# Attention, the order within a step: TensorE turns four tiles before the next scores, VectorE copies them before it adds the bias

## The chip, the core and the metric

The kernel runs on one core of one Trainium2 chip. The metric is the device time in microseconds of one execution; lower is better. The kernel before took 1315.04 us, the median of three executions (1312.54, 1315.04 and 1316.11).

## The reference, cut to what matters

```python
def _attn_ref(q, k, v, w1, b1, w2):          # q, k, v: 4 x 8 x 576 x 64, float32
    scores = np.matmul(q, k.transpose(0, 1, 3, 2)) / np.sqrt(D)
    ...                                       # bias: a table 576 x 576 for each of 8 heads
    scores = scores + bias.transpose(2, 0, 1)[None, :, :, :]
    scores = scores - np.max(scores, axis=-1, keepdims=True)
    attn = np.exp(scores)
    attn = attn / (np.sum(attn, axis=-1, keepdims=True) + 1e-09)
    return np.matmul(attn, v)
```

Behind it stand a dense layer (2304 tokens, 512 to 2048 to 512, with h - tanh(h) between) and a layer of 8 experts, of which each token goes to the one with the largest gate. All tensors are float32.

## The kernel before, in words

The program has five blocks, one after the other: `bias_tables`, `attention`, `dense_layer`, `routing` and `experts`. Only `attention` is touched.

It works on 16 pairs of heads, g = 0 to 15. A head has 576 queries, in QT = 5 tiles: t = 0 to 3 have 128 rows, t = 4 has 64. The list `STEPS` holds all (g, t) in order, with five steps ahead of the first pair and five behind the last; n = 5 g + t numbers a pair's tiles. Each engine goes through the same list with its own instructions, written out by hand. A step does several jobs on different tiles at once, and semaphores hold the engines together. In step n:

- TensorE (from line 396): `scores` of tile n+1 (line 341) multiplies q by k for both heads c = 0 and 1, as three products of split numbers (high by high, high by low, low by high), in two halves of 288 keys: 12 matmuls. Then four transposes of the probabilities of tile n into the bank `pt_a` (line 404, through `turn_prob`, line 355), then products with v (`values_main`, lines 407 to 410: one slot in step 4, and of the pair before one slot, two slots and one slot in steps 0, 1 and 2, none in step 3), then four transposes into `pt_b` (line 415). Then come transposes of the next pair's q and k (line 430; steps 0 to 3), in step 2 the last 64 queries' products with v (line 423), in steps 3 and 4 transposes of the output `o_sb` (line 439), and one last transpose of tile n, `mid`, into the bank `misc` (line 444).
- VectorE (from line 518): `add_bias` of tile n+1 for both heads (line 487): it reads the scores and the bias, writes the negated sum `neg` and its row minimum `negmax`. Then the copy of `pt_a` into `prob_t` (line 529), then the low parts of the next pair's k and q (lines 536 and 539), and, for the pair before: the reciprocal of the sums in step 1, two copies into `o_sb` in step 2 (lines 551 and 555), the scaling into `x_sb` in steps 3 and 4 (line 511).
- ScalarE (from line 459): the exponential of tile n+1 of head 0 (line 454), the copy of `pt_b` (line 472), the copy of `mid` (line 474), the high parts of the next pair's k and q (line 479), the exponential of tile n+1 of head 1.
- SP loads q, k, v and the bias, and stores `x_sb` to `x_dram`.

Each engine works strictly in the order of its list. What matters here: `scores` of tile n+1 waits until both bias additions of tile n have read its banks (line 343); the `pt_a` transposes of tile n wait for that tile's exponential of head 0 (`prob_done[0]`, line 401) and for VectorE's copy of tile n-1 (`pta_read`, line 403); the `pt_b` transposes wait for the exponential of head 1 (line 412). An exponential waits for its own `add_bias` (line 451). The `o_sb` copy of the remainder waits for ScalarE's `mid` copy (line 554).

Of the kernel before, what the change touches and what calls it, by code (L numbers as in the profile page):

```python
# [30 lines left out]
QT = -(-S // P)  # L31
# [13 lines left out]
def rows(t):  # L45

    return P if t < QT - 1 else LAST
# [149 lines left out]
def attention(nc, bias_dram, q, k, v, ident, x_dram):  # L197
# [6 lines left out]
    with ExitStack() as ctx:  # L204
# [58 lines left out]
        def q_at(t):  # L263

            return 0 if t == QT - 1 else LAST + t * P
# [14 lines left out]
        def real(g):  # L280
            return 0 <= g < PAIRS_A
# [3 lines left out]
        with nc.Block() as block:  # L285
# [49 lines left out]
            @block.tensor  # L335
            def _(pe):
                def scores(g, t):
                    n = g * QT + t
                    if t == 0 or NEEDED[t] > NEEDED[t - 1]:
                        pe.wait_ge(lo_done, NP * g + NEEDED[t])  # L340
                    for c in range(2):
                        if n:
                            pe.wait_ge(neg_done[c], n)
                    cols = slice(q_at(t), q_at(t) + P)
                    for half in range(2):
                        keys = slice(half * HALF, (half + 1) * HALF)
                        for i, (a, b) in enumerate(((q_hi, k_hi), (q_hi, k_lo), (q_lo, k_hi))):
                            for c in range(2):
                                part = slice(c * D, (c + 1) * D)
                                last = nc.tensor.matmul(score[c][:, half, 0:HALF], a[g % 2][part, cols], b[g % 2][part, keys],  # L350
                                                        start=i == 0, stop=i == 2)
                                if half and i == 2:
                                    last.then_inc(score_done[c], 1)

                def turn_prob(bank, at, n, j):
                    m = rows(n % QT)
                    src = prob[n % 2][0:m, :, :].rearrange("p c s -> p (c s)")[:, j * P:(j + 1) * P]
                    return nc.tensor.transpose(bank[:, at:at + m], src, id_sb[0:m, 0:m])

                def values(g, slot, o, at, queries):  # L360

                    j_a, j_b = (slot, MID + 1 + slot) if slot < MID else (MID, MID)
                    for c, j in ((0, j_a), (1, j_b)):
                        keys = slice(0, P) if j != MID else slice(c * D, (c + 1) * D)
                        last = nc.tensor.matmul(o[c * D:(c + 1) * D, at:at + queries.stop - queries.start],  # L365
                                                v_nat[g % NV][keys, j, :], prob_t[g % 2][keys, j, queries],
                                                start=slot == 0, stop=slot == MID)
                    return last

                def values_main(g, slots):  # L370
                    if 0 in slots:
                        pe.wait_ge(v_in[g % NV], 16 * (g // NV + 1))
                        pe.wait_ge(pta_read, QT * g + QT - 1)
                        pe.wait_ge(ptb_read, QT * g + QT - 1)
                        pe.wait_ge(mid_read, QT * g + QT - 1)
                        if g:
                            pe.wait_ge(o_read, g)
                    for slot in slots:
                        last = values(g, slot, o_acc, 0, slice(0, MAIN))
                    if MID in slots:  # L380
                        last.then_inc(o_done, 1)

                def misc_free(g, t):

                    pg, pt = (g, t - 1) if t else (g - 1, QT - 1)
                    if real(pg):
                        pe.wait_ge(mid_read, QT * pg + pt + 1)
                    if pt < NP and real(pg + 1):
                        pe.wait_ge(lo_done, NP * (pg + 1) + pt + 1)
                    if pt == 2 and real(pg - 1):  # L390
                        pe.wait_ge(rem_read, pg)
                    if pt >= 3 and real(pg - 1):
                        pe.wait_ge(x_done, 2 * (pg - 1) + pt - 2)

                pe.wait_ge(id_in, 16)
                for g, t in STEPS:
                    n = g * QT + t
                    if real((n + 1) // QT):
                        scores((n + 1) // QT, (n + 1) % QT)
                    if real(g):  # L400
                        pe.wait_ge(prob_done[0], n + 1)
                        if n:
                            pe.wait_ge(pta_read, n)
                        for j in range(MID):
                            last = turn_prob(pt_a, j * P, n, j)
                        last.then_inc(pta_done, 1)
                    if t == QT - 1 and real(g):
                        values_main(g, (0,))
                    if t < 3 and real(g - 1):
                        values_main(g - 1, ((1,), (2, 3), (4,))[t])  # L410
                    if real(g):
                        pe.wait_ge(prob_done[1], n + 1)
                        if n:
                            pe.wait_ge(ptb_read, n)
                        for j in range(MID + 1, KTP):
                            last = turn_prob(pt_b, (j - MID - 1) * P, n, j)
                        last.then_inc(ptb_done, 1)
                    misc_free(g, t)
                    if t == 2 and real(g - 1):
                        pe.wait_ge(pta_read, QT * g)  # L420
                        pe.wait_ge(ptb_read, QT * g)
                        pe.wait_ge(mid_read, QT * g)
                        for slot in range(MID + 1):
                            last = values(g - 1, slot, misc, REM, slice(MAIN, S))
                        last.then_inc(rem_done, 1)
                    if t < NP and real(g + 1):
                        if t == 0:
                            pe.wait_ge(qk_in[(g + 1) % NQK], 128 * ((g + 1) // NQK + 1))
                        at = P
                        for x, tile, m in PIECES[t]:  # L430
                            nat = (k_nat if x == "k" else q_nat)[(g + 1) % NQK]
                            last = nc.tensor.transpose(misc[:, at:at + m], nat[0:m, tile, :], id_sb[0:m, 0:m])
                            at += m
                        last.then_inc(prep_done, 1)
                    if t in TURNED and real(g - 1):
                        pe.wait_ge(o_read, g)
                        if t == 4:
                            pe.wait_ge(rem_read, g)
                        for tile, at in TURNED[t]:
                            m = rows(tile)  # L440
                            last = nc.tensor.transpose(misc[0:m, at:at + P], o_sb[:, tile * P:tile * P + m], id_sb[:, :])
                        last.then_inc(turn_done, 1)
                    if real(g):
                        turn_prob(misc, 0, n, MID).then_inc(mid_done, 1)
# [41 lines left out]
            def _(dve):  # L486
# [31 lines left out]
                for g, t in STEPS:  # L518
                    n = g * QT + t
                    m = rows(t)  # L520
                    if real((n + 1) // QT):
                        add_bias(n + 1, 0)
                        add_bias(n + 1, 1)
                    if real(g):
                        if t == 0 and g >= 2:
                            dve.wait_ge(rem_done, g - 1)
                        dve.wait_ge(pta_done, n + 1)
                        src = pt_a[:, :].rearrange("p (k m) -> p k m", m=P)
                        nc.vector.tensor_copy(prob_t[g % 2][:, 0:MID, t * P:t * P + m], src[:, :, 0:m]).then_inc(pta_read, 1)
                    if t < NP and real(g + 1):  # L530
                        i = (g + 1) % 2
                        dve.wait_ge(hi_done, NP * (g + 1) + t + 1)
# [1046 lines left out]
```

## Time and profile before

| | us |
|---|---|
| median of three executions | 1315.04 |
| the profiled execution | 1314.88 |
| its span, first to last instruction | 1312.9 |
| TensorE matmul, busy | 1078.8 (82%) |
| VectorE, busy | 710.6 (54%) |
| ScalarE, busy | 567.5 (43%) |
| bias additions, line 496, 160 of them, busy | 113.9 |
| exponentials, line 454, 160 of them, busy | 124.2 |

The profile is of one execution. The hardware profiler's times are microseconds from the first instruction unless marked ns. PE is TensorE's matmuls, PEld its weight loads, DVE VectorE, ACT ScalarE. A busy time can contain time in which a matmul only drains, since ends of matmuls are modelled: a matmul's start after the one before it says more than its duration. The attention's first instructions start at 72 us, its last ends at 419 us.

### The profile page before, as it was taken

To read this page: it belongs to the slowest core of one execution; us is meant where nothing else is said; L and a number is where in the kernel's file an instruction comes from. 1 tells how busy PE (TensorE), PEld (TensorE's weight loads), DVE (VectorE), ACT (ScalarE), POOL (GpSimd) and SP (SyncE) were. 2 spreads that over 40 slices of the span, in tenths; PEclk is the share of its full clock that TensorE was granted. 3 is DMA by queue.
4 is the path that set the end of the run, shared out by engine and by line. 5 is a ranking of instruction groups with operands and counts; after the bars stand their busy time and mean duration, and the time that the engine had idled before them with its cause. 6 is when DMAs were issued, how large, how long until landed. Compare 5 with 4: busy or idle time off the path is not lost. (4 is left out here: it accounts for less than half of the span.)

```text
span 1312.9 us, 19829 instructions
## 1 busy us (share of the span) xinstructions
PE 1078.8 (82%) x6632; PEld 822.5 (63%) x6632; DVE 710.6 (54%) x1515; ACT 567.5 (43%) x1181; POOL 88.5 (7%) x132
## 2 busy tenths in 40 slices
PE   4755999999996689999999899993603998999995
PEld 2233666666663578888888788882302777777773
DVE  6933766766764587676666667671322245242320
ACT  4733666666663454444443444440213144242320
POOL 0000000000000000000000000000062221222221
PEclk9967999999998799999999999996956999999997
DMA  3587222222212420000000100004073326121010
GB/s 112 200 240 221 55 65 64 60 60 65 66 26 65 174 97 25 25 25 25 24 24 0 46 3 0 24 0 174 0 162 91 127 76 235 48 92 48 29 40 29
DMA packets 106822, 96.54 MB, mean 74 GB/s; under 512 B 63475, under 2 KB 73523, under 8 KB 106740
## 3 DMA queue, kind: packets, MB, share of 16 engines
q1 hardware_dynamic: 102564, 84.73, 21.3%
q0 software_dynamic: 4176, 10.80, 2.6%
q8 instruction: 41, 0.67, 0.2%
q14 instruction: 41, 0.34, 0.1%
HBM read 70.71 MB, written 25.61 MB: 73 GB/s over the span
## 5 line engine op out<-in xcount | busy, mean ns | idle before, releaser
L454 ACT ACTIVATE at_prob<-at_neg,at_negmax 128x576 f32<-128x576 f32 (+1 forms) x160 | 124.2, 777 | 63.9 <-DVE at_negmax L496 54.7
L719 PE MATMUL dl_x_ps<-dl_wout_hi,dl_g_hi 128*128 128x512 f32 x288 | 115.9, 402 | 32.5 <-DVE dl_g_lo L954 32.5
L709 PE MATMUL dl_h_ps<-dl_xt_hi,dl_win_hi 128*128 128x384 f32 x384 | 131.7, 343 | 1.4 <-DVE dl_xt_lo L889 1.4
L709 PE MATMUL dl_h_ps<-dl_xt_hi,dl_win_lo 128*128 128x384 f32 x384 | 130.2, 339 | 0.0
L709 PE MATMUL dl_h_ps<-dl_xt_lo,dl_win_hi 128*128 128x384 f32 x384 | 129.9, 338 | 0.0
L496 DVE CUSTOM_DVE_ANT_0 at_neg<-at_score,at_bias 128x576 f32<-128x576 f32 (+1 forms) x160 | 113.9, 747 | 7.8 <-PE at_score L350 7.8
L719 PE MATMUL dl_x_ps<-dl_wout_lo,dl_g_hi 128*128 128x512 f32 x288 | 114.5, 398 | 0.0
L719 PE MATMUL dl_x_ps<-dl_wout_hi,dl_g_lo 128*128 128x512 f32 x288 | 114.5, 397 | 0.0
L790 ACT ACTIVATE dl_val<-dl_h_ps 128x384 f32<-128x384 f32 x93 | 45.7, 491 | 126.9 <-PE dl_h_ps L709 106.8
L719 PEld LDWEIGHTS dl_x_ps<-dl_wout_hi,dl_g_hi 128*128 128x128 f32 x288 | 54.4, 189 | 49.4 <-DVE dl_g_lo L954 31.8
L1315 POOL DMA_INDIRECT slot_dram<-slot_rows,slot_i x18 | 19.8, 1102 | 962.7 <-POOLq L1059 957.5
L365 PE MATMUL at_o_acc<-at_prob_t,at_v_nat 128*64 128x512 f32 (+1 forms) x320 | 83.1, 615 | 0.1
L1476 DVE TENSOR_TENSOR ex_ht_lo<-ex_ht_ps,ex_ht_hi 128x512 fp32r<-128x512 f32 x42 | 27.1, 686 | 102.0 <-ACT ex_ht_hi L1432 102.0
L709 PEld LDWEIGHTS dl_h_ps<-dl_xt_hi,dl_win_hi 128*128 128x128 f32 x384 | 73.1, 190 | 5.3 <-DVE dl_xt_lo L889 1.8
L709 PEld LDWEIGHTS dl_h_ps<-dl_xt_lo,dl_win_hi 128*128 128x128 f32 x384 | 73.0, 190 | 3.4
L1358 PE MATMUL ex_xt_ps<-ex_id_sb_e,ex_x_sb_e 128*128 128x128 f32 x88 | 15.1, 297 | 70.4 <-DMA ex_x_sb_e<-x_dram,ex_rows_g 70.4
L709 PEld LDWEIGHTS dl_h_ps<-dl_xt_hi,dl_win_lo 128*128 128x128 f32 x384 | 72.8, 189 | 0.0
L1367 PE MATMUL ex_h_ps_e<-ex_w_hi,ex_xt_hi_e 128*128 128x512 f32 x168 | 69.8, 416 | 3.6 <-DVE ex_xt_lo_e L1476 3.6
L1387 PE MATMUL ex_y_ps<-ex_w_hi,ex_ht_hi 128*128 128x512 f32 (+1 forms) x168 | 69.4, 413 | 0.9 <-issue 0.9
L350 PE MATMUL at_score<-at_k_hi,at_q_hi 64*128 64x288 f32 x320 | 58.8, 349 | 12.3 <-DVE at_negmax L496 12.3
L1367 PE MATMUL ex_h_ps_e<-ex_w_lo,ex_xt_hi_e 128*128 128x512 f32 x168 | 67.8, 403 | 0.0
L1367 PE MATMUL ex_h_ps_e<-ex_w_hi,ex_xt_lo_e 128*128 128x512 f32 x168 | 67.5, 402 | 0.0
(155 smaller groups left out, 2301.5 us busy)
## 6 DMA issues: line engine op xcount, KB each, us to landing
ex_raw<-in_moe_w SPq DMA_DIRECT2D x20, 1024.0 KB, 6.6
bias_dram<-bt_rows_sb SPq DMA_DIRECT2D x36, 288.0 KB, 2.1
at_bias<-bias_dram SPq DMA_DIRECT2D x8, 1152.0 KB, 10.6
at_v_nat<-in_v SPq DMA_DIRECT2D x16, 288.0 KB, 3.0
dl_x_nat<-x_dram SPq DMA_DIRECT2D x6, 768.0 KB, 4.6
x_dram<-dl_x_sb SPq DMA_DIRECT2D x6, 768.0 KB, 3.5
rt_x_all<-x_dram SPq DMA_DIRECT2D x6, 768.0 KB, 8.6
at_k_nat<-in_k SPq DMA_DIRECT2D x32, 128.0 KB, 2.4
```

Of the source, the lines that this page charges most:

```text
L350: last = nc.tensor.matmul(score[c][:, half, 0:HALF], a[g % 2][part, cols], b[g % 2][part, keys], start=i == 0, stop=i == 2)
L365: last = nc.tensor.matmul(o[c * D:(c + 1) * D, at:at + queries.stop - queries.start], v_nat[g % NV][keys, j, :], prob_t[g % 2][keys, j, qu ...
L454: nc.scalar.activation(prob[n % 2][0:m, c, :], neg[c][n % 2][0:m, :], ACT.Exp, bias=negmax[c][n % 2][0:m, 0:1], scale=-1.0, accum_out=tota ...
L496: nc.vector.tensor_tensor_reduce(out=neg[c][n % 2][0:m, :].rearrange("p (a c) -> p a c", a=2), in0=score[c][0:m, :, 0:HALF], in1=bias[0:m, ...
L709: last = nc.tensor.matmul(h_ps[slot % NHB][:, 0:CN], w[:, k, fc], x[k2][:, k, :], start=k == 0 and n == 0, stop=k == KT - 1 and n == 2)
L719: last = nc.tensor.matmul(x2_ps[j][:, :], g[p2][:, tok], w[:, f, :], start=f == 0 and n == 0, stop=f == FT - 1 and n == 2)
L790: nc.scalar.activation(val[p2][:, :], h_ps[slot % NHB][:, 0:CN], ACT.Square).then_inc(act_step, 1)
L1315: nc.gpsimd.indirect_dma_start(slot_dram, bass.IndirectOffsetOnAxis(ap=slot_i[:, t:t + 1], axis=0), rows_sb[:, t, :], None).then_inc(scatt ...
L1358: last = nc.tensor.transpose(xt_ps[:, k, :], x_sb[:, k * P:(k + 1) * P], id_sb[:, :])
L1367: last = nc.tensor.matmul(h_ps[half][:, :], x[:, k, :], w[:, e % 2, k, half_cols(half)], start=k == 0 and n == 0, stop=k == KT - 1 and n == 2)
L1387: last = nc.tensor.matmul(y_ps[:, :], x[:, k, :], of_set(w, k), start=k == 0 and n == 0, stop=k == EK - 1 and n == 2)
L1476: nc.vector.tensor_tensor(out, full, high.bitcast(F32), ALU.subtract).then_inc(done, 1)
```

## The change

TensorE's scores of the next tile move behind the four `pt_a` transposes of this tile. VectorE's two bias additions of the next tile move behind the `pt_a` copy of this tile. Nothing else differs; waits move with the instructions they belong to.

```diff
@@ -395,8 +395,6 @@
                 pe.wait_ge(id_in, 16)
                 for g, t in STEPS:
                     n = g * QT + t
-                    if real((n + 1) // QT):
-                        scores((n + 1) // QT, (n + 1) % QT)
                     if real(g):
                         pe.wait_ge(prob_done[0], n + 1)
                         if n:
@@ -404,6 +402,8 @@
                         for j in range(MID):
                             last = turn_prob(pt_a, j * P, n, j)
                         last.then_inc(pta_done, 1)
+                    if real((n + 1) // QT):
+                        scores((n + 1) // QT, (n + 1) % QT)
                     if t == QT - 1 and real(g):
                         values_main(g, (0,))
                     if t < 3 and real(g - 1):
@@ -518,15 +518,15 @@
                 for g, t in STEPS:
                     n = g * QT + t
                     m = rows(t)
-                    if real((n + 1) // QT):
-                        add_bias(n + 1, 0)
-                        add_bias(n + 1, 1)
                     if real(g):
                         if t == 0 and g >= 2:
                             dve.wait_ge(rem_done, g - 1)
                         dve.wait_ge(pta_done, n + 1)
                         src = pt_a[:, :].rearrange("p (k m) -> p k m", m=P)
                         nc.vector.tensor_copy(prob_t[g % 2][:, 0:MID, t * P:t * P + m], src[:, :, 0:m]).then_inc(pta_read, 1)
+                    if real((n + 1) // QT):
+                        add_bias(n + 1, 0)
+                        add_bias(n + 1, 1)
                     if t < NP and real(g + 1):
                         i = (g + 1) % 2
                         dve.wait_ge(hi_done, NP * (g + 1) + t + 1)
```

## Rows read from the trace of the kernel before

**Rows 1.** The page, the span in 40 slices: granted clock of TensorE in tenths

```profile
PEclk9967999999998799999999999996956999999997
```

**Rows 2.** Busy time by stretch: length; PE, PEld, DVE, ACT, POOL busy; clock; DMA share, GB/s

```profile
143.67:396.00 252.33, 243.03 (x2085) 155.40 (x2081) 174.34 (x484) 167.84 (x457) 0.00 (x0) 1.00 0.25 59
```

**Rows 3.** Waits of TensorE, 125 to 405 us: total, times, longest

```profile
PE at_score L350 <- DVE at_negmax L496: 10.0, 14, 0.7
```

**Rows 4.** Timeline, TensorE, steps 1 to 3: start, time until the last's end

```profile
300.21 0.40 PE L350 MATMUL at_score<-at_k_hi,at_q_hi 64*128 64x288 f32 x2
...
301.20 0.66 PE L358 MATMUL at_pt_a<-at_id_sb,at_prob 128*128 128x128 f32 x4
...
301.78 1.94 PE L365 MATMUL at_o_acc<-at_prob_t,at_v_nat 128*64 128x512 f32 x8
...
309.50 0.40 PE L350 MATMUL at_score<-at_k_hi,at_q_hi 64*128 64x288 f32 x2
...
310.49 0.66 PE L358 MATMUL at_pt_a<-at_id_sb,at_prob 128*128 128x128 f32 x4
...
310.98 0.64 PE L358 MATMUL at_pt_b<-at_id_sb,at_prob 128*128 128x128 f32 x4
...
311.84 0.27 PE L358 MATMUL at_misc<-at_id_sb,at_prob 128*128 128x128 f32 x1
```

**Rows 5.** Timeline, TensorE, step 4 and the start of step 0

```profile
312.83 0.40 PE L350 MATMUL at_score<-at_k_hi,at_q_hi 64*128 64x288 f32 x2 [0.71 <-DVE at_negmax L496]
...
313.69 0.40 PE L358 MATMUL at_pt_a<-at_id_sb,at_prob 64*128 64x64 f32 x4
...
315.91 0.45 PE L350 MATMUL at_score<-at_k_hi,at_q_hi 64*128 64x288 f32 x2
```

**Rows 6.** Timeline, TensorE, end of step 0 and start of step 1

```profile
319.36 0.27 PE L358 MATMUL at_misc<-at_id_sb,at_prob 128*128 128x128 f32 x1
...
319.56 0.40 PE L350 MATMUL at_score<-at_k_hi,at_q_hi 64*128 64x288 f32 x2
```

**Rows 7.** Timeline, VectorE, steps 2 to 0

```profile
306.71 0.74 DVE L496 CUSTOM_DVE_ANT_0 at_neg<-at_score,at_bias 128x576 f32<-128x576 f32 x1
...
310.53 0.68 DVE L551 COPY at_o_sb<-at_o_acc 128x512 f32<-128x512 f32 x1
311.13 0.21 DVE L555 COPY at_o_sb<-at_misc 128x64 f32<-128x64 f32 x1
311.26 0.74 DVE L496 CUSTOM_DVE_ANT_0 at_neg<-at_score,at_bias 64x576 f32<-64x576 f32 x1
...
313.74 0.29 DVE L539 SCALAR_TENSOR_TENSOR at_q_lo<-at_misc,at_q_hi 128x128 fp32r<-128x128 f32 x1 [0.45 <-ACT at_q_hi L479]
...
314.28 0.75 DVE L496 CUSTOM_DVE_ANT_0 at_neg<-at_score,at_bias 128x576 f32<-128x576 f32 x1
...
315.63 0.42 DVE L529 COPY at_prob_t<-at_pt_a 128x256 f32<-128x256 f32 x1
...
317.07 0.74 DVE L496 CUSTOM_DVE_ANT_0 at_neg<-at_score,at_bias 128x576 f32<-128x576 f32 x1
```

**Rows 8.** Timeline, TensorE, in step 0 of pair 1

```profile
123.31 0.87 PE L432 MATMUL at_misc<-at_id_sb,at_k_nat 128*128 128x128 f32 x3 [14.85 <-DMA at_q_nat<-in_q]
```

**Rows 9.** Timeline, TensorE, the dense layer's first instruction

```profile
426.64 1.08 PE L700 MATMUL dl_turn<-dl_id_sb_d,dl_x_nat 128*128 128x128 f32 x4 [8.86 <-DMA dl_x_nat<-x_dram]
```

**Rows 10.** Timeline, ScalarE, the first exponential of tile 4

```profile
312.04 0.77 ACT L454 ACTIVATE at_prob<-at_neg,at_negmax 64x576 f32<-64x576 f32 x1 [1.13 <-DVE at_negmax L496]
```

**Rows 11.** Timeline, pair 0: an exponential, and transposes that waited for it

```profile
97.30 0.79 ACT L454 ACTIVATE at_prob<-at_neg,at_negmax 128x576 f32<-128x576 f32 x1
...
98.23 0.66 PE L358 MATMUL at_pt_b<-at_id_sb,at_prob 128*128 128x128 f32 x4 [0.25 <-ACT at_prob L454]
```

**Rows 12.** Timeline, TensorE, step 4 of the last pair

```profile
408.39 0.43 PE L358 MATMUL at_pt_a<-at_id_sb,at_prob 64*128 64x64 f32 x4 [0.87 <-DVE at_prob_t L529]
```

**Rows 13.** Instructions of tile `at_score`: duration in ns, min/median/max

```profile
L350 PE MATMUL at_score<-at_k_hi,at_q_lo x320: 285/288/439, 86.0 to 405.9; 64*128 64x288 f32 x160
```

## The prediction

> **What bounds the kernel now.** I read the clock slices first. The granted clock is full through the attention's steady stretch and lower at its start [rows 1]. The busy time by stretch says why order matters there: from 143.67 to 396.00 us TensorE is busy 243.03 of 252.33 us, 96% [rows 2]. So the attention runs at TensorE's pace, and time is gained or lost only where TensorE's queue stands still. The waits of TensorE show one such place: 14 waits, 10.0 us in all, each of at most 0.7 us, by the score matmuls for VectorE's `negmax` [rows 3].
>
> The timeline shows where it lies. A pair of heads has five steps; I call them by t. Step 1 begins with its scores at 300.21, step 3 at 309.50, step 4 at 312.83, step 0 of the next pair at 315.91, and its step 1 at 319.56 [rows 4 to 6]. The pair repeats every 319.56 - 300.21 = 19.35 us. Steps 1 and 2 have 9.29 us of TensorE work, step 0 has 3.65. Step 3 is short: its last transpose starts at 311.84, and the next scores could go about 0.2 later, at 312.04, but start at 312.83. VectorE is late there: it had to copy `o_sb` (310.53, 311.13) before it could begin the bias additions of tile 4 at 311.26 [rows 4, 5, 7].
>
> What reaches the end: a delay before 123 us does not, since TensorE then stands 14.85 us for `q_nat` by DMA [rows 8]. That transfer (of pair 2, counted from 0) is queued on SP behind the bias loads, and waits for no step of pair 0 or 1; it covers all of pair 0. A delay after it does reach the end: the dense layer's first transpose waits for `x_dram`, which the attention's last store writes [rows 9]. I count the pairs from 1 to 14, one for each wait of [rows 3], and treat the last pair apart.
>
> **The change, part by part.** Nothing is added or removed; two things swap places on two engines. TensorE's step is now: four `pt_a` transposes (tile n), scores (n+1), values, the rest. VectorE's is: `pt_a` copy (n), two bias additions (n+1), the rest. No DMA is issued by either moved part; SP waits for the prepared tiles, the remainder and `x_done`, all a whole pair ahead of their use.
>
> First, what now stands at the head of a step. Before, the scores (n+1) needed both bias additions (n). Now the transposes of tile n need its first exponential, one ScalarE instruction further on, and the scores stand behind them. Latencies along this loop: scores' start to bias addition 317.07 - 315.91 = 1.16; bias addition to exponential 312.04 - 311.26 = 0.78; exponential to the transposes it feeds 98.23 - 97.30 = 0.93 [rows 5, 7, 10, 11]. With the transposes ahead of the scores (0.58, from 301.20 to 301.78 [rows 4]) a step can't now be shorter than 0.58 + 1.16 + 0.78 + 0.93 = 3.45 us. Steps 1 and 2 are far above it and step 0 (3.65) just above. Step 3 has 312.04 - 309.50 = 2.54 us of work, step 4 has 315.91 - 312.83 = 3.08 [rows 4, 5]. They are where it costs.
>
> Second, VectorE's copy. It takes 0.68 us and its successor can start 0.60 after it, as after the `o_sb` copy of the same length (310.53 to 311.13 [rows 7]). It now stands ahead of the bias additions, so wherever VectorE has a backlog they start 0.60 later.
>
> Working through step 3. VectorE reaches the point of 311.26 as before, since all that leads there (the split of q, the `o_sb` copies) hangs on step 2. It copies `pt_a` until 311.86, then adds the bias of tile 4; the exponential starts at 312.64, and the transposes of step 4 at 313.57. Before, step 4 began at 312.83. TensorE has been out of work since about 312.04, so its wait grows from 0.8 to about 1.5 us, and step 4 begins 0.74 late.
>
> Working through step 4. From first exponential to VectorE's `q_lo` took 313.74 - 312.04 = 1.70, as ScalarE's copies stand between; so `q_lo` goes to 312.64 + 1.70 = 314.34. It and the scaling take 314.28 - 313.74 = 0.54, until 314.88; the short `pt_a` copy (0.42 long, 0.34 to its successor) until 315.22 [rows 7, 10]. The scores are no tighter bound: 313.57 + 0.34 + 1.16 = 315.07, the 0.34 being four 64-row transposes (here the row at 313.69 to the values). So the bias of the next tile 0 starts at 315.22, its exponential at 316.00, and step 0 at 316.93. TensorE's own work would let it go at 313.57 + 3.08 = 316.65, a little more with the last transpose. Before, step 0 began at 315.91. Steps 3 and 4 together: 7.43 in place of 6.41, **+1.02 us a pair**.
>
> Cover in the other steps. In step 2 the bias addition was at 306.71 [rows 7]; with the copy ahead 307.31, exponential 308.09, transposes possible at 309.02, before TensorE arrives at 309.50: hidden with 0.48 to spare (0.30 if the gains below are taken off). In step 0 the loop of 3.45 stands against 3.65: hidden with 0.20 to spare. If that cover went, each 0.1 would cost 1.4 us over the 14 pairs. Second exponentials and `pt_b` keep their order and their feeders.
>
> Third, a gain. A change between transposing and multiplying costs TensorE something: four transposes to the next four take 310.98 - 310.49 = 0.49, but 0.58 to the values that follow at 301.78; and the last transpose of a step leads the scores by 319.56 - 319.36 = 0.20, where one transpose among others takes 0.12 [rows 4, 6]. So 0.08 to 0.09 a change. Before, a step with values had transpose, scores, transpose, values: three changes. After: transposes next to transposes, scores, values: two, of which scores to values is a kind that no row shows. It can cost nothing (multiplying both times) or as much as the others, or more. I take 0.09, as both neighbours have it: one change saved, 0.09 in each of steps 1, 2 and 0. Step 3, without values, keeps two changes; step 4 is bound by the chain. **-0.27 us a pair.** At the other end (free) it is 0.18 in steps 1 and 2 and in step 0 no more than its cover of 0.20: 0.54 in all. With nothing gained, 0.
>
> The last pair: its step 4 has no scores behind it and waited 0.87 us for VectorE's `pt_a` copy [rows 12]. That wait ends earlier now but the exponential comes later; with small gains in its other steps I put it at nothing, within 0.5 us either way.
>
> **Sum.** 1.02 - 0.27 = 0.75 a pair, times 14 = +10.5 us. The profiled execution took 1314.88 us (span 1312.9), so 1325.4. That execution is 0.16 below the median of three, 1315.04, which needs no correction. Ends: no gain from fewer changes, 14 x 1.02 = +14.3, 1329.2; the largest gain, 14 x 0.48 = +6.7, 1321.6. Each latency is a difference of two rows and may be off by some hundredths; 0.1 in the chain of steps 3 and 4 is 1.4 us.
>
> A rule weighed: from 131 to 394 us every slice shows the full clock [rows 1], and from 143.67 to 396.00 it is 1.00 [rows 2], with TensorE idle in spells of up to 0.8 us a pair. The Trainium skill, in TensorE: Matmul & The Clock Gate, section "A second HAM failure mode: psum-queue depth-cycling", says that brief but frequent idling between groups of matmuls can make the clock swing between its levels. It speaks against this change, which doubles the spell to 1.5 us. By that rule the sum would be that of the second rival below. The trace before does not bear it out at 0.8 us a pair; no row shows 1.5 us in this pattern.
>
> **Rivals.** (a) *The swap pays.* TensorE's wait for `negmax` (10.0 us) vanishes, because the transposes fill it and the exponential is there in time. Then steps 3 and 4 shrink by 0.79 and the changes give 0.27 or more: -1.06 a pair, -15 us, 1300. It decides at step 4's first transpose: it must start by about 312.1, at the latest before 312.83 for a gain. For it: the wait of the scores does end earlier relative to them. Against it: bias addition (311.26 at best), 0.78 and 0.93 alone give 312.97, even with no copy ahead. Even then one saved change a step makes it a small gain at most. 4%.
>
> (b) *The clock falls* in the longer wait of step 3, at a pair's step 4. At the lower level (1.2 GHz) a score matmul takes up to 439 ns against 288 [rows 13], 1.52 times. If step 0 (3.65 us) ran so, it would add 1.9 us a pair, 27 us, about 1352. For it: the wait doubles. Against it: TensorE stays busy in all else. 4%.
>
> (c) *Nothing measurable*: the saved changes are worth far more than 0.09, about 0.25 a step, and give back all but 0.28 a pair: under +3.9 us, below 1318.8. For it: scores and values may overlap in the array in a way that no row shows. Against it: step 0 can't take more than 0.20. 8%. That the change doesn't take effect can be left out: both lists are written out by hand in the order of issue.
>
> **How the numbers follow.** The forecast's mechanism has 84%, with 1325.4 as its value. About 0.3% is what a measurement of this kernel can tell from no change, 3.9 us. The range reaches from 1318.5 (largest gain and a chain 0.2 shorter) to 1331 (no gain and a chain 0.1 longer); it leaves out (a), (b) and the lower part of (c). Slower: 84 + 4 = 88%; same 8%; faster 4%.
>
> **What would show it.** After the change the 14 waits of the scores are gone, and the first `pt_a` transpose of each step 4 waits for ScalarE's `at_prob`, 14 times about 1.3 to 1.5 us, some 20 us in all. A pair takes 20.1 us, steps 3 and 4 7.4 of it; steps 1 and 2 take 9.1; the clock stays full; the dense layer starts some 10 us later and the stages behind it take what they took. It is wrong if the pair stays at or below 19.6 us, if the wait in step 4 is under 1 us, or if step 0 waits too, for a bias addition behind the scalings of step 4.

## The result and the profile after

The changed kernel takes 1327.14 us (median of 8), the kernel before 1316.09 in the same comparison (median of 8). The ratio is 1.0087 with a 95% interval from 1.0068 to 1.0107: slower by 0.87%, which is 11.4 us of the median before; the two medians themselves lie 11.05 us apart. Forecast were 10.5 us. The profiled execution took 1327.18 us, with a span of 1324.7.

Of the page after, the granted clock of TensorE in 40 slices, in answer to [rows 1]:

```profile
PEclk9968999999999699999999999997955999999997
```

A 9 only says 90% or more, so the steady stretch needs a row of its own. Busy time by stretch, after (length; PE, PEld, DVE, ACT, POOL; clock; DMA share, GB/s), in answer to [rows 2]:

```profile
131.00:413.00 282.00, 261.24 (x2245) 167.72 (x2241) 188.90 (x524) 179.07 (x490) 0.00 (x0) 1.00 0.23 55
```

From 131 to 413 us the clock is 1.00, as before, and TensorE is busy 93% of the time. Counting the slices from 0, slice 13 (430 to 464 us) holds most of the pause between the attention and the dense layer and that layer's start; before, they fell in slices 12 and 13. The waits of TensorE from 125 to 420 us (total, times, longest), in answer to [rows 3]:

```profile
PE at_pt_a L358 <- ACT at_prob L454: 21.0, 15, 1.4
PE at_o_acc L365 <- ACT at_prob_t L474: 0.4, 1, 0.4
```

The 14 waits of the scores, 10.0 us, are gone. In their place the transposes wait for the exponential, 15 times (14 pairs and the last), up to 1.4 us. The timeline of TensorE over one pair, in answer to [rows 4 to 6]:

```profile
305.62 0.60 PE L358 MATMUL at_pt_a<-at_id_sb,at_prob 128*128 128x128 f32 x4
306.15 0.40 PE L350 MATMUL at_score<-at_k_hi,at_q_hi 64*128 64x288 f32 x2
...
306.91 0.29 PE L350 MATMUL at_score<-at_k_hi,at_q_lo 64*128 64x288 f32 x2
307.13 1.94 PE L365 MATMUL at_o_acc<-at_prob_t,at_v_nat 128*64 128x512 f32 x8
...
310.24 0.60 PE L358 MATMUL at_pt_a<-at_id_sb,at_prob 128*128 128x128 f32 x4
...
314.50 0.27 PE L358 MATMUL at_misc<-at_id_sb,at_prob 128*128 128x128 f32 x1
314.61 0.60 PE L358 MATMUL at_pt_a<-at_id_sb,at_prob 128*128 128x128 f32 x4
...
317.05 0.27 PE L358 MATMUL at_misc<-at_id_sb,at_prob 128*128 128x128 f32 x1
318.76 0.34 PE L358 MATMUL at_pt_a<-at_id_sb,at_prob 64*128 64x64 f32 x2 [1.44 <-ACT at_prob L454]
...
322.18 0.66 PE L358 MATMUL at_pt_a<-at_id_sb,at_prob 128*128 128x128 f32 x4
...
325.58 0.27 PE L358 MATMUL at_misc<-at_id_sb,at_prob 128*128 128x128 f32 x1
325.69 0.60 PE L358 MATMUL at_pt_a<-at_id_sb,at_prob 128*128 128x128 f32 x4
```

A step now begins with its `pt_a` transposes: step 1 at 305.62, step 2 at 310.24, step 3 at 314.61, step 4 at 318.76, step 0 at 322.18, the next step 1 at 325.69. The pair takes 20.07 us in place of 19.35. Read against the steps of before:

| | before | after | forecast |
|---|---|---|---|
| steps 1 and 2 | 9.29 | 8.99 | 9.11 |
| steps 3 and 4 | 6.41 | 7.57 | 7.43 |
| step 0 | 3.65 | 3.51 | 3.56 |
| a pair | 19.35 | 20.07 | 20.10 |

The timeline of VectorE, steps 3 and 4, in answer to [rows 7], and of ScalarE, its two exponentials, in answer to [rows 10]:

```profile
316.33 0.22 DVE L555 COPY at_o_sb<-at_misc 128x64 f32<-128x64 f32 x1
316.46 0.68 DVE L526 COPY at_prob_t<-at_pt_a 128x512 f32<-128x512 f32 x1
317.06 0.74 DVE L496 CUSTOM_DVE_ANT_0 at_neg<-at_score,at_bias 64x576 f32<-64x576 f32 x1
...
320.08 0.42 DVE L526 COPY at_prob_t<-at_pt_a 128x256 f32<-128x256 f32 x1
320.42 0.75 DVE L496 CUSTOM_DVE_ANT_0 at_neg<-at_score,at_bias 128x576 f32<-128x576 f32 x1
```

```profile
317.84 0.77 ACT L454 ACTIVATE at_prob<-at_neg,at_negmax 64x576 f32<-64x576 f32 x1 [1.73 <-DVE at_negmax L496]
...
321.26 0.78 ACT L454 ACTIVATE at_prob<-at_neg,at_negmax 128x576 f32<-128x576 f32 x1 [0.98 <-issue]
```

This is the chain of the forecast, link by link: `o_sb` copies, `pt_a` copy at 316.46, bias 0.60 later, exponential 0.78 later, transposes 0.92 later at 318.76, while TensorE had nothing to do after about 317.25.

**The whole attention.** 14 times 0.72 is 10.1 us. The first transpose of the dense layer comes at 437.57 in place of 426.64 [rows 9], 10.93 later. Between these two numbers lie several things on either side of the 14 pairs, which in part cancel. The last transpose of step 3 comes at 136.44 in place of 137.62 in pair 1, 1.18 earlier, and at 416.29 in place of 407.25 in the last pair, 9.04 later: 10.22 us over 14 pairs, as the pairs say.

Of the 1.18 us at the start, 0.17 are there at the last transpose of step 0 (123.80 in place of 123.97), since the transfer of [rows 8] landed earlier. Steps 1 and 2 give 0.15 each, as in every pair. The other 0.71, all in step 1, came with the clock, which rose sooner. Busy time by stretch, before and after:

```profile
125.00:130.00 5.00, 5.00 (x27) 2.62 (x25) 2.60 (x6) 1.71 (x5) 0.00 (x0) 0.70 0.26 59
```

```profile
125.00:130.00 5.00, 5.00 (x34) 3.21 (x33) 2.55 (x6) 2.30 (x6) 0.00 (x0) 0.88 0.21 46
```

In the second profile of the changed kernel, e9 below, the same five microseconds have a clock of 0.57, so the earlier rise is no part of the change.

The last pair. TensorE there, before (beside [rows 12]):

```profile
410.83 4.14 PE L365 MATMUL at_o_acc<-at_prob_t,at_v_nat 128*64 128x512 f32 x16
414.90 0.95 PE L365 MATMUL at_misc<-at_prob_t,at_v_nat 128*64 128x64 f32 x20
```

and after:

```profile
417.40 0.46 PE L358 MATMUL at_pt_a<-at_id_sb,at_prob 64*128 64x64 f32 x4 [0.83 <-ACT at_prob L454]
418.27 1.08 PE L365 MATMUL at_o_acc<-at_prob_t,at_v_nat 128*64 128x512 f32 x4 [0.41 <-ACT at_prob_t L474]
...
420.76 4.98 PE L365 MATMUL at_o_acc<-at_prob_t,at_v_nat 128*64 128x512 f32 x16
425.67 0.95 PE L365 MATMUL at_misc<-at_prob_t,at_v_nat 128*64 128x64 f32 x20
```

Its step 4 begins 9.01 us later than before, its last values begin 9.93 later (420.76 against 410.83), and what follows them 10.77 later; the last 0.16 to the dense layer lie in the store and load of `x_dram`. A wait of 0.41 us is new: these values need ScalarE's copy of `mid` of step 3, which stands behind the late exponential, and here no scores lie between. And the 16 values take 4.91 us to the next instruction in place of 4.07, because the clock fell. Busy time by stretch, after (length; PE, PEld, DVE, ACT, POOL; clock; DMA share, GB/s):

```profile
419.00:420.00 1.00, 1.00 (x8) 0.65 (x7) 0.00 (x0) 0.22 (x1) 0.00 (x0) 0.88 0.00 0
420.00:421.00 1.00, 1.00 (x6) 0.50 (x6) 0.00 (x0) 0.30 (x2) 0.00 (x0) 0.50 0.00 0
...
423.00:424.00 1.00, 1.00 (x6) 0.28 (x4) 0.00 (x0) 0.00 (x0) 0.00 (x0) 0.92 0.71 210
```

From late in 419 to early in 423 us the granted clock is 0.50, that is 1.2 GHz, after a stretch in which TensorE had waited 0.83 and 0.41 us. Slice 12 of the page (397 to 430 us) reads 9 all the same, since its mean is 0.95. Experiment e9 asks whether the fall recurs.

### The profile page after: what moved, and what is told of

Read it like the earlier page. It is cut to its first block and busy times, and to the rows that moved or that the text cites. A ratio compares the mean times of both kernels' runs of the same rounds, so it can differ in the third digit from the quotient of the medians.

```text
span 1324.7 us, 19829 instructions
## 1 busy us (share of the span) xinstructions
PE 1081.6 (82%) x6632; PEld 824.1 (62%) x6632; DVE 711.3 (54%) x1515; ACT 566.4 (43%) x1181; POOL 88.9 (7%) x132
## 5 line engine op out<-in xcount | busy, mean ns | idle before, releaser
L358 PE MATMUL at_pt_a<-at_id_sb,at_prob 128*128 128x128 f32 (+1 forms) x320 | 48.2, 274 | 26.2 <-ACT at_prob L454 25.7
## 6 DMA issues: line engine op xcount, KB each, us to landing
at_bias<-bias_dram SPq DMA_DIRECT2D x8, 1152.0 KB, 10.5
```

## The experiments

Two theories were open behind the number. The forecast's: the price lies in steps 3 and 4 alone, where a loop over the engines and VectorE's backlog bind, and a gain lies in the other steps. Against it stood that one half of the change alone (VectorE's copy ahead of the bias, or TensorE's transposes ahead of the scores) carries the price, and that the price is spread over all steps. All ratios below are against the kernel before on the same chip, with 95% intervals; the change in us is the ratio less one, times the median of before in the same comparison.

| | ratio (95%) | us | a pair |
|---|---|---|---|
| full change | 1.0087 (1.0068 to 1.0107) | +11.4 | 20.07 |
| e1, TensorE's half | 1.0096 (1.0078 to 1.0114) | +12.6 | 20.21 |
| e2, VectorE's half | 1.0135 (1.0118 to 1.0153) | +17.8 | 20.52 |
| e3, steps 3 and 4 only | 1.0095 (1.0079 to 1.0111) | +12.5 | 20.20 |
| e4, steps 0, 1, 2 only | 0.9983 (0.9971 to 0.9996) | -2.2 | 19.28 |
| e5, TensorE, steps 1 and 2 | 0.9959 (0.9944 to 0.9974) | -5.4 | 19.06 |
| e6, before, `o_sb` on ScalarE | 0.9940 (0.9924 to 0.9957) | -7.9 | 18.76 |
| e7, full change, `o_sb` on ScalarE | 1.0015 (1.0002 to 1.0028) | +2.0 | 19.47 |
| e8, e5 and e6 | 0.9911 (0.9894 to 0.9928) | -11.7 | 18.46 |

The last column is the distance between the same instruction in two neighbouring pairs of the timeline, for a pair like most of the 14; single pairs that take longer are named with their run.

### e1 and e2: each half alone

```diff
 # e1, against the full change: VectorE as before
+                    if real((n + 1) // QT):
+                        add_bias(n + 1, 0)
+                        add_bias(n + 1, 1)
                     if real(g):
...
-                    if real((n + 1) // QT):
-                        add_bias(n + 1, 0)
-                        add_bias(n + 1, 1)
```

> Only TensorE's half of the change; VectorE adds the bias first and copies pt_a second, as before. Theory (the loop from one step's transposes to the next is what binds): the copy, now behind two bias additions, releases pt_a late. In step 4 the transposes wait for VectorE's copy of step 3: 312.61 + 0.83 = 313.44 on the scale of the kernel before, hardly earlier than in the full change; and step 0 becomes a loop of 0.53 + 1.16 + 1.36 (two bias additions) + 0.83 (copy to transposes) = 3.9 us in place of 3.5. A pair takes about 20.35 us, 1.0 more than before: +14 us, slower than the full change by some 3 to 4 us. Rival (VectorE's copy ahead of the bias is what costs 0.6 in step 3): without it a pair takes about 19.5, the kernel is 8 us faster than the full change and within 3 us of before.

The waits of TensorE in e1, and its timeline with VectorE's copy:

```profile
PE at_pt_a L358 <- DVE at_prob_t L529: 21.5, 28, 1.3
```

```profile
318.51 0.68 DVE L529 COPY at_prob_t<-at_pt_a 128x512 f32<-128x512 f32 x1
```

```profile
319.34 0.43 PE L358 MATMUL at_pt_a<-at_id_sb,at_prob 64*128 64x64 f32 x4 [1.32 <-DVE at_prob_t L529]
...
326.50 0.63 PE L358 MATMUL at_pt_a<-at_id_sb,at_prob 128*128 128x128 f32 x4 [0.20 <-DVE at_prob_t L529]
```

The transposes of step 4 wait for the copy, 0.83 us from its start (318.51 to 319.34), not for the exponential. And step 0 has become longer too: step 1's transposes at 326.50 wait as well, so 28 waits. The pair takes 326.50 - 306.29 = 20.21 us. In the full change VectorE's new order avoids just that, so it is no cost of its own there: without it the kernel is no faster. How much slower it is was forecast too high: 3 to 4 us were expected, the pairs give 0.14 times 14, 2 us, and by the times the two kernels can't be told apart (12.6 against 11.4 us, with intervals of some 2 us either way).

```diff
 # e2, against the full change: TensorE as before
+                    if real((n + 1) // QT):
+                        scores((n + 1) // QT, (n + 1) % QT)
                     if real(g):
...
-                    if real((n + 1) // QT):
-                        scores((n + 1) // QT, (n + 1) % QT)
```

> Only VectorE's half; TensorE issues the scores first, as before. Theory: the bias addition now waits for the pt_a transposes that stand behind the scores and for the copy: about 2.35 us from the scores' start to it, in place of 1.16, and the next scores wait for both bias additions: a loop of 3.9 us a step. Step 3 loses 0.6, step 4 0.3, step 0 0.3: +1.2 us a pair, 20.5, +16 us in all, all of it as waits of the scores for negmax. Rival (TensorE's half alone costs, because the transposes wait for the exponential): this one stays within 3 us of before.

```profile
PE at_score L350 <- DVE at_negmax L496: 22.4, 28, 1.3
```

The waits of before have grown from 10.0 us in 14 to 22.4 in 28, and the pair is 20.52 where 20.5 was expected. The rival, that VectorE's half costs nothing by itself, falls. With TensorE issuing scores first, a bias addition waits for transposes and a copy that it has no need of. So it is not one half that brings the price into the full change: each half costs at least as much by itself as both do together, and what stays with both is the longer loop.

### e3 and e4: the short steps and the long steps

```diff
 # e3; e4 the same with (0, 1, 2). VectorE's add_bias is split in the same way
+                    if t not in (3, 4) and real((n + 1) // QT):
+                        scores((n + 1) // QT, (n + 1) % QT)
                     if real(g):
...
-                    if real((n + 1) // QT):
+                    if t in (3, 4) and real((n + 1) // QT):
                         scores((n + 1) // QT, (n + 1) % QT)
```

> The full change, but in steps 3 and 4 alone; steps 0, 1, 2 keep the order of before. Theory: the whole cost and none of the gain: 4.26 us from the last transpose of step 2 to step 4, then 3.24 to the scores of step 0, 7.50 in place of 6.61: +0.9 us a pair, about 20.25, +12.5 us. Rival (the cost is spread over all steps): less than half of that, under +6.

> The full change, but in steps 0, 1 and 2 alone; steps 3 and 4 keep the order of before. Theory: the gain without the cost: steps 1 and 2 shorter by 0.15 each, step 0 waits about 0.14 for its exponential and gains as much; a pair of 19.1 in place of 19.35, -3 us in all, near the limit of what can be measured; the 14 waits of the scores for negmax in step 4 stay as before (10 us). Rival (a saved change between transposing and multiplying is worth nothing, and the shorter steps of the full change come from elsewhere): 0 or slower.

Waits and two neighbouring pairs in e3:

```profile
PE at_pt_a L358 <- ACT at_prob L456: 20.2, 14, 1.4
```

```profile
301.17 0.33 PE L358 MATMUL at_pt_a<-at_id_sb,at_prob 64*128 64x64 f32 x2 [1.45 <-ACT at_prob L456]
...
321.37 0.34 PE L358 MATMUL at_pt_a<-at_id_sb,at_prob 64*128 64x64 f32 x2 [1.44 <-ACT at_prob L456]
```

The new order in two of five steps costs what the whole change costs, with the same 14 waits. In e4 the waits are those of before:

```profile
PE at_score L350 <- DVE at_negmax L498: 10.0, 14, 0.7
```

and the kernel is a little faster. The pair is 19.28, 0.18 longer than the 19.1 expected: from the last transpose of step 4 to the next tile's it takes 0.29 us there (314.46 to 314.75), not about 0.15. The exponential is not what it waits for: started at 313.67, it would let the transposes go at 314.60. VectorE's copy of step 4 fits: in e4 it stands behind the bias additions, starts at 314.18 and is 0.42 long, and the longer copy in e1 let the transposes go 0.15 after its end, which gives 314.75. This is read from the distances and was not tried.

The two ratios multiplied give 1.0078, against 1.0087 for the full change; by the pairs, +0.85 and -0.07 make 0.78 against 0.72. So price and gain about add up, and they lie where the forecast put them.

### e5: the gain alone

```diff
+                    if t not in (1, 2) and real((n + 1) // QT):
+                        scores((n + 1) // QT, (n + 1) % QT)
                     if real(g):
...
+                    if t in (1, 2) and real((n + 1) // QT):
+                        scores((n + 1) // QT, (n + 1) % QT)
```

> TensorE's new order in steps 1 and 2 alone, VectorE and all other steps as before. Theory: steps 1 and 2 give 0.15 us each and wait for nothing (their exponentials and copies are done 0.5 us and more ahead): a pair of 19.05, -0.3, -4 to -5 us in all. The 14 waits for negmax stay. Rival (VectorE's order is needed for the gain): the copy of pt_a now comes late and steps 1 or 2 wait for at_prob_t.

It is faster than the kernel before, by 0.41%. The pair is 19.06: 317.42 against 298.36 for the last transpose of step 0. The waits are those of e4, with none new. So VectorE's order has no part in the gain of steps 1 and 2.

### e6 and e7: VectorE's backlog ahead of step 4

The large copy into `o_sb` (0.68 us on VectorE, just ahead of the bias of tile 4) goes to ScalarE, behind its last exponential of step 2. VectorE keeps the small one.

```diff
 # ScalarE, at the end of a step
+                    if t == 2 and real(g - 1):
+                        if g > 1:
+                            act.wait_ge(turn_done, 2 * (g - 1))
+                        act.wait_ge(o_done, g)
+                        nc.scalar.activation(o_sb[:, 0:MAIN], o_acc[:, :], ACT.Copy).then_inc(o_read, 1)
 # VectorE
-                            dve.wait_ge(o_done, g)
-                            nc.vector.tensor_copy(o_sb[:, 0:MAIN], o_acc[:, :]).then_inc(o_read, 1)
```

> The kernel before, with the large copy into o_sb moved from VectorE to ScalarE, behind its last exponential of step 2. Theory (VectorE's backlog there is what TensorE waits for in step 4): the bias addition of tile 4 starts 0.6 us earlier, bound by the scores' end; the 14 waits of 0.71 fall to 0.2 or less; a pair of 18.75, -8 to -9 us in all. Rival (ScalarE's copy is as late, or holds up the exponential or the transposes of o_sb): the wait moves to the transposes in step 3, and less than 3 us are gained.

> The full change with the same move of the o_sb copy. Theory (the price of the change is backlog plus loop latency): the backlog's 0.6 goes, the loop's latency stays: the waits of the transposes for the exponential fall from 1.44 to about 0.9, a pair of 19.5, +1 to +2 us against before. Rival (the latency of the loop alone sets steps 3 and 4): nothing changes against the full change, +11.

The waits in e6:

```profile
PE at_score L350 <- DVE at_negmax L501: 2.7, 14, 0.3
```

10.0 us of waits became 2.7, and the time fell by 7.9 us: the wait of before was VectorE's backlog. The waits in e7, and its VectorE around step 3:

```profile
PE at_pt_a L358 <- ACT at_prob L454: 13.7, 15, 1.0
```

```profile
309.36 0.21 DVE L558 COPY at_o_sb<-at_misc 128x64 f32<-128x64 f32 x1
309.49 0.68 DVE L531 COPY at_prob_t<-at_pt_a 128x512 f32<-128x512 f32 x1
310.09 0.74 DVE L501 CUSTOM_DVE_ANT_0 at_neg<-at_score,at_bias 64x576 f32<-64x576 f32 x1
```

The wait of step 4 fell from 1.44 to 0.91 us, not to nothing: with the backlog taken away the loop's own latency stays. The change costs 0.75% (1.0015 against 0.9940) on top of e6, and 0.71 us a pair, nearly as much as on top of before. The pair is 19.47, as expected. Of the pairs 2 to 14 two take longer, pair 3 with 19.60 and pair 11 with 19.65. The last transpose of step 4 in pairs 9, 10 and 11, and VectorE's scaling into `x_sb` in step 0 of pairs 10 and 11:

```profile
295.43 0.27 PE L358 MATMUL at_misc<-at_id_sb,at_prob 64*128 64x64 f32 x1
...
314.89 0.27 PE L358 MATMUL at_misc<-at_id_sb,at_prob 64*128 64x64 f32 x1
...
334.54 0.27 PE L358 MATMUL at_misc<-at_id_sb,at_prob 64*128 64x64 f32 x1
```

```profile
296.17 0.61 DVE L516 TENSOR_TENSOR at_x_sb<-at_misc,at_inv 128x256 f32<-128x256 f32 x2 [0.76 <-ACT at_prob_t L474]
...
315.99 0.61 DVE L516 TENSOR_TENSOR at_x_sb<-at_misc,at_inv 128x256 f32<-128x256 f32 x2 [1.11 <-ACT at_prob_t L474]
```

The scaling at 315.99 is 0.36 us late against the one a pair before, and the `pt_a` copy and the bias addition stand behind it. The cover of step 0 is thin in this kernel: with the exponential at 298.21 the transposes could go at 299.14, and TensorE is ready for them at 299.24. A delay of 0.36 uses it up, and step 1 of pair 11 is 0.18 longer. Why the scaling is late was not found.

### e8: the two gains together

> The o_sb copy on ScalarE and TensorE's new order in steps 1 and 2. Theory: both gains add, as they lie in different steps: a pair of 18.45, -13 us in all, about 1304. Rival: they share the same slack (the shorter step 2 leaves VectorE later in step 3), and the sum is under -10.

This is the fastest version: 1303.29 us, 0.89% under the kernel before. By the times -5.4 and -7.9 would be -13.3 and measured are -11.7, with an interval that holds both (-13.9 to -9.5). By the pairs the gains add fully: 0.29 and 0.59 off 19.35 give 18.47. The last transpose of step 4 in pairs 9, 10 and 11:

```profile
287.63 0.27 PE L358 MATMUL at_misc<-at_id_sb,at_prob 64*128 64x64 f32 x1
...
306.09 0.27 PE L358 MATMUL at_misc<-at_id_sb,at_prob 64*128 64x64 f32 x1
...
324.72 0.27 PE L358 MATMUL at_misc<-at_id_sb,at_prob 64*128 64x64 f32 x1
```

Pair 10 takes 18.46, as do all of the pairs 2 to 14 but two, and 18.45 was expected. Pair 11 takes 18.63 and pair 3 18.61, the same two that are longer in e7, and in pair 11 the scaling is 0.35 us late here too. Together they are 0.3 us. So the rival, a shared slack, shows nothing in the steady pairs.

### e9: the change once more

> The full change once more, unaltered, to see what in its profile recurs. Theory (the clock's fall in the last pair is a matter of the moment, the pair's schedule is fixed by the program): a pair takes 20.07 again and the 14 waits are 1.44 us each; the 16 values of the last pair take 4.14 us, as with a full clock, in place of 4.98. Rival (the waits of step 4 in the last pair bring the clock down each time): 4.98 again, with the clock at half for some 3 us before and within it.

One execution: 1326.04 us, span 1323.9. TensorE in a steady pair and in the last one:

```profile
300.62 0.34 PE L358 MATMUL at_pt_a<-at_id_sb,at_prob 64*128 64x64 f32 x2 [1.44 <-ACT at_prob L454]
...
320.71 0.33 PE L358 MATMUL at_pt_a<-at_id_sb,at_prob 64*128 64x64 f32 x2 [1.45 <-ACT at_prob L454]
...
420.23 1.08 PE L365 MATMUL at_o_acc<-at_prob_t,at_v_nat 128*64 128x512 f32 x4 [0.38 <-ACT at_prob_t L474]
...
422.30 4.14 PE L365 MATMUL at_o_acc<-at_prob_t,at_v_nat 128*64 128x512 f32 x16
```

The pair (20.09 between these rows) and its wait recur. The fall of the clock in the last pair does not: the 16 values take 4.14 us, with the same waits of 0.83 and 0.38 us ahead of them. So the fall is an affair of one execution and no fixed part of the 11.4 us. The new wait for ScalarE's copy recurs. The two executions give the price of each. From the transposes of the last step 4 to the values of the remainder, before took 6.51 us (408.39 to 414.90), e9 6.99 (419.38 to 426.37) and the changed kernel's first profile 8.27 (417.40 to 425.67): 0.48 for the new wait and what hangs on it, 1.28 for the fall of the clock.

## Why the prediction was right

**The place.** That attention runs at TensorE's pace and that the price lies in steps 3 and 4 was right: with the new order there alone (e3) the kernel loses as much as with the full change, and without it there (e4) it loses nothing.

**The chain.** From the last transpose of step 2, on which all hangs, the forecast gave 4.27 us to step 4 (309.30, the start of that transpose in the kernel before, to 313.57), measured are 318.76 - 314.50 = 4.26. From step 4 to step 0 it gave 3.36, measured 3.42: of the 0.06, all lies between bias addition and exponential of the next tile 0 (320.42 to 321.26, 0.84, where 0.78 was taken from another tile). That the backlog and the loop's latency are both in it is shown by e7: without 0.6 us of backlog the wait goes from 1.44 to 0.91.

**The gain.** The forecast took 0.09 in each of three steps. Measured are 0.15, 0.15 and 0.14. The term was too small, for a reason that no row of before showed: not only does the step's last transpose lead into the next without a change (314.50 to 314.61, 0.11 in place of 0.20), the four transposes of such a run also hand over sooner (305.62 to 306.15, 0.53 in place of 0.58). In step 0, where they come after a short standstill, they don't (322.18 to 322.76, 0.58); there the scores take 0.99 in place of the 1.03 of before, and why was not followed. The unknown change, scores to values, costs what the other changes cost: 306.91 to 307.13 is 0.22 from the last pair of scores to the values, where neighbours among the scores are about 0.13 apart. The value taken for it, 0.09, was right. Of step 2's gain 0.09 is given back at once, as step 3 starts earlier and waits longer; that is why steps 3 and 4 read 7.57 rather than 7.48.

Put together: a price of 1.07 (forecast 1.02), a gain of 0.35 (forecast 0.27), 0.72 a pair (forecast 0.75), 10.1 us over 14 pairs (forecast 10.5). Two small errors cancel, which is luck. The split is read from the rows of the full change. Run apart, its parts are smaller, 0.85 a pair in e3 and 0.07 in e4, since the seam between steps 4 and 0 falls otherwise in each: step 0 of e3 begins with scores, which don't wait for the exponential, and step 0 of e4 waits 0.29 us.

**What the forecast left out.** In the last pair it expected nothing within 0.5 us. Its step 4 does come as the 14 pairs say (9.01 later, its own wait 0.83 in place of 0.87), but the wait of the values for ScalarE's copy, which no term had, makes it 0.48. The clock, which it took as full, did two things outside the steady stretch of this execution: it rose sooner in pair 1 (0.71 us gained) and fell in the last pair (1.28 lost). They cancel in part; without both, the dense layer's 10.93 would be 10.36. The rest of the program added 0.9 us to the span after the dense layer's start; with runs of one kernel spread over 8 us this was not followed.

**The rivals.** (a), the swap pays, is gone: step 4's transposes began 1.71 us after the last of step 3, not at once; e5 shows the version in which it does pay, where nothing waits. (c), saved changes worth 0.25 a step, is refuted by 0.15. (b), the clock: from 131 to 413 us the granted clock is 1.00 with 1.44 us of waiting in each pair of 20 us, so the swing between levels, which the Trainium skill names for brief and frequent idling (TensorE: Matmul & The Clock Gate, "A second HAM failure mode: psum-queue depth-cycling"), did not come. The single fall, in the last pair of one of two profiles of this kernel, cost 1.28 us, 0.84 of it at the 16 values.

## What to carry to other kernels

When two engines hand work back and forth, write down for each step the shortest loop (here transposes, scores, bias, exponential: 3.45 us) and compare it with the work that the bound engine has in that step: an order is good for the long steps and bad for the short ones, and it can be chosen for each step. Swap an order on one engine only after asking what the other engine now releases late; e2, one half alone, was some 6 us slower than both together, and e1, the other half, no faster. Before changing an order to fill a wait, look at what is queued ahead of the releasing instruction: moving one 0.68 us copy to an engine with room (e6) gave more than any order did.

## What the runs showed of the hardware that was not expected

A run of transposes behind transposes gave way to the scores 0.53 us after the start of the last four (305.62 to 306.15), against 0.58 to the values for four transposes behind a product [rows 4] and 0.58 to the scores for four transposes after a short standstill (322.18 to 322.76). And the clock fell to 1.2 GHz once, from late in 419 to early in 423 us, in stretches in which TensorE was fully busy, after waits of 0.83 and 0.41 us; the same program with the same waits kept the full clock in another execution, and 14 waits of 1.44 us did not bring it down in either. Its rise at the start of pair 1, after a wait for a transfer, varies from one execution to the next as well: from 125 to 130 us the mean is 0.70 in the kernel before, 0.88 and 0.57 in two executions of the changed one.
